# A small constant as a ninth row, one relu remainder moved behind a balancing chain, and six tile scalings on ScalarE

## The reference

```python
logits = x @ w_gate
logits = logits - logits.max()
P = np.exp(logits)
for _ in range(8):
    P /= P.sum(1, keepdims=True) + 1e-09     # over the 8 experts of a token
    P /= P.sum(0, keepdims=True) + 1e-09     # over all 2304 tokens of an expert
    P *= N / E
out = np.zeros((N, D), dtype=np.float32)
for e in range(E):
    h = np.maximum(x @ w1[e], 0.0)
    ye = h @ w2[e]
    out += P[:, e:e + 1] * ye
```

## Time and profile before

| what | value |
|---|---|
| median of three runs | 1865.8 us |
| the profiled execution's own time | 1865.84 us |
| its span, first to last instruction | 1864.0 us |
| PE, share of the span busy | 99% |
| VectorE, ScalarE, GpSimd busy | 58%, 44%, 55% |
| PE idle between 382 and 490 us (108.00 long, 101.09 busy) | 6.91 us |
| PE idle from 490 us to the end (1374.00 long, 1369.93 busy) | 4.07 us |

### The profile page before, as it was taken

One profiled execution on the slowest core, in us unless ns is written; L12 is line 12 of the kernel. 1 busy time (PEld: TensorE's weight loads), 2 busy tenths in 40 slices (PEclk: granted clock), 3 DMA queues, 4 the chain that ended last, 5 costly groups with the idle time before them and its releaser, 6 DMA issues.

```text
span 1864.0 us, 28112 instructions
## 1 busy us (share of the span) xinstructions
PE 1841.2 (99%) x10255; PEld 1594.7 (86%) x10255; DVE 1072.5 (58%) x1846; ACT 815.6 (44%) x1410; POOL 1027.8 (55%) x720
## 2 busy tenths in 40 slices
PE   8999999999999999999999999999999999999999
PEld 4677777788899999999999999999999999999998
DVE  8877777778845554556455545554555455545553
ACT  8777767533333333334333343333333333333331
POOL 0223226476666666665776666666665666666661
PEclk9999999999999999999999999999999999999999
DMA  7763552111111211112211211122122111111110
GB/s 245 221 150 87 131 144 54 46 68 69 47 69 69 69 68 69 68 69 99 72 69 69 70 68 70 69 69 70 70 94 76 69 69 68 70 69 69 69 51 34
DMA packets 44163, 152.57 MB, mean 82 GB/s; under 512 B 9594, under 2 KB 18042, under 8 KB 29710
## 3 DMA queue, kind: packets, MB, share of 16 engines
q1 hardware_dynamic: 44046, 151.04, 25.1%
HBM read 135.69 MB, written 15.34 MB: 81 GB/s over the span
## 4 chain that ended last, share of the span: by engine, by line
PE 94%; DVE 4%; ACT 1%; issue 1%; DMA 0%; DVEq 0%; SPq 0%; ACTq 0%
PE banks L673 13%; PE banks L674 13%; PE banks L672 13%; PE banks L640 12%; PE banks L644 12%; PE banks L642 12%; PE banks L555 4%; PE banks L516 3%; PE banks L498 3%; PE banks L464 2%; PE banks L499 2%; DVE h_lo L1173 1%; PE banks L581 1%; DVE routing L1129 0%; PE banks L526 0%
## 5 line engine op out<-in xcount | busy, mean ns | idle before, releaser
L1283 POOL TENSOR_TENSOR w_lo<-stage,w_hi 128x1024 fp32r<-128x1024 f32 (+1 forms) x288 | 646.8, 2260 | 539.8 <-ACT w_hi L842 538.1
L1167 DVE TENSOR_TENSOR u<-p_copy,banks 128x384 f32<-128x384 f32 x192 | 106.4, 554 | 632.3 <-PE banks L644 632.2
L674 PE MATMUL banks<-w_hi,h_lo 128*128 128x512 f32 x1152 | 450.1, 391 | 0.0
L673 PE MATMUL banks<-w_lo,h_hi 128*128 128x512 f32 x1152 | 449.9, 391 | 0.0
L672 PE MATMUL banks<-w_hi,h_hi 128*128 128x512 f32 x1152 | 448.9, 390 | 0.0
L1173 DVE SCALAR_TENSOR_TENSOR h_lo<-corner,h_hi 128x384 fp32r<-128x384 f32 x384 | 408.1, 1091 | 0.0
L889 ACT ACTIVATE h_hi<-corner 128x384 fp32r<-128x384 f32 x384 | 196.6, 526 | 272.5 <-DVE corner L1167 269.3
L640 PE MATMUL banks<-x_hi,w_hi 128*128 128x384 f32 x896 | 301.1, 336 | 4.9 <-DVE u L1167 2.4
L644 PE MATMUL banks<-x_hi,w_lo 128*128 128x384 f32 x896 | 300.2, 335 | 0.0
L842 ACT ACTIVATE w_hi<-stage 128x1024 fp32r<-128x1024 f32 (+1 forms) x288 | 271.7, 974 | 7.9 <-POOL stage L1277 7.9
L878 ACT ACTIVATE p_copy<-banks 128x384 f32<-128x384 f32 x96 | 47.3, 492 | 503.7 <-PE banks L644 503.7
(11 more groups left out here) (135 smaller groups left out, 2501.4 us busy)
## 6 DMA issues: line engine op xcount, KB each, us to landing
stage<-in_expert_w SPq DMA_DIRECT2D x96, 1024.0 KB, 4.7
raw<-in_qk SPq DMA_DIRECT2D x32, 576.0 KB, 7.2
bias_scratch<-bias_out SPq DMA_DIRECT2D x36, 288.0 KB, 2.8
bias<-bias_scratch SPq DMA_DIRECT2D x16, 288.0 KB, 2.8
v_main<-in_v SPq DMA_DIRECT2D x16, 256.0 KB, 2.7
bias<-bias_scratch SPq DMA_DIRECT2D x16, 256.0 KB, 3.8
out<-total SPq DMA_DIRECT2D x4, 768.0 KB, 3.9
out<-total SPq DMA_DIRECT2D x6, 256.0 KB, 2.0
```

The lines of the kernel that those rows point to most:

```text
L673: pe.matmul(dst, h_hi[:, g % 2, f, tokens], lo[:, f], start=False, stop=False)
L674: mm = pe.matmul(dst, h_lo[:, g % 2, f, tokens], hi[:, f], start=False, stop=fp == FPAIRS - 1 and f == 1)
L1167: dve.tensor_tensor(out, other, bank, op).then_inc(combined, 1)
L1283: pool.tensor_tensor(lo, of, hi.bitcast(F32), ALU.subtract).then_inc(w_split, 1)
```

## The change

There are four edits. First, a buffer `weighed` of nine rows of 18 takes the place of `routing`, which becomes a view of its first eight rows; the ninth row holds 1e-9, written once at the start. The sums over the experts now add nine rows, and the separate addition of the constant goes. Second, in periods with a total at place 4 (2, 3, 5 and 6) split 3 moves from ahead of the second chain to behind it. Third, the six scalings of the first expert's tiles move from VectorE to ACT, behind its last weight rounding of period 7; ACT waits there for the last column scaling (`balanced`). Fourth, the spreading of the largest logit moves on PE from behind token block 5 of period 1 to behind block 4.

```diff
-        routing = sb("routing", [P, E, TOK])
+        weighed = sb("weighed", [P, E + 1, TOK])
+        routing = weighed[:, 0:E]
...
-        TOP_ALL = (1, 5)
+        TOP_ALL = (1, 4)
...
+            def scale_first(j):
+
+                act.wait_ge(balanced, 1)
+                act.wait_ge(y_added, j + 1)
+                act.activation(total[:, j, :], total[:, j, :], ACT.Copy,
+                               scale=tile_weight(0, 0, j)).then_inc(first_scaled, 1)
...
+                if g == TOTALS[-1][0]:
+                    for j in range(TJ):
+                        scale_first(j)
...
             dve.memset(ones[:], 1.0).then_inc(ones_set, 1)
+            dve.memset(weighed[:, E], EPS).then_inc(eps_set, 1)
...
                 if k == 0:
+                    dve.wait_ge(eps_set, 1)
                     dve.wait_ge(exp_ready, 1)
-                link(dve.tensor_reduce(sums[:], routing[:].rearrange("p e c -> p c e"), AX_X, ALU.add))
-                link(dve.tensor_scalar(sums[:], sums[:], EPS, None, ALU.add))
+                link(dve.tensor_reduce(sums[:], weighed[:].rearrange("p e c -> p c e"), AX_X, ALU.add))
                 link(dve.reciprocal(inverse[:], sums[:]))
...
+                if k < ITERS - 1:
+                    link(scaled_columns)
+                else:
+                    scaled_columns.then_inc(balanced, 1)
...
-            def scale_first(j):
-
-                dve.wait_ge(y_added, j + 1)
-                dve.tensor_scalar(total[:, j, :], total[:, j, :], tile_weight(0, 0, j), None,
-                                  ALU.mult).then_inc(first_scaled, 1)
...
-                if g == 2 * FPAIRS - 2:
-                    scale_first(j)
...
                     if expert == 1:
+                        dve.wait_ge(balanced, 1)
                         dve.wait_ge(first_scaled, j + 1)
...
-                split_hidden(g, 3)
+                if (g, 4) not in TOTALS:
+                    split_hidden(g, 3)
                 add_tile(g - 1, 2)
                 for j in range(3, TJ):
                     read_side(g, j)
                     add_tile(g - 1, j)
+                if (g, 4) in TOTALS:
+                    split_hidden(g, 3)
```

More of the change, by code:

```diff
@@ L232, in bass_attention_moe @@
         first_scaled = sem("first_scaled")
+        balanced = sem("balanced")
+        eps_set = sem("eps_set")
         top_all = sem("top_all")
@@ L312, in first_low, with tile_weight @@
             return x_lo_first[:, k] if k < EARLY else x_lo_rest[:, k - EARLY]
+        def tile_weight(p, e, j):
+            return routing[:, e, TJ * p + j:TJ * p + j + 1]
         def high_part(p, k):
@@ L908, in place_logits @@
                 turned = banks[:, TURNED_BANK, :]
-                to = routing[:].rearrange("p e (j q) -> p q j e", q=T // P)
+                to = routing.rearrange("p e (j q) -> p q j e", q=T // P)
                 first = turned[:, 0:3 * P].rearrange("p (q j r) -> p q j r", q=T // P, r=C)
@@ L937, in _ @@
                     act.wait_ge(top_neg, 1)
-                    act.activation(routing[:], routing[:], ACT.Exp, bias=top[:, 1:2]).then_inc(exp_ready, 1)
+                    act.activation(routing, routing, ACT.Exp, bias=top[:, 1:2]).then_inc(exp_ready, 1)
                 if after == 1:
@@ L1104, in largest_logit @@
                 dve.wait_ge(logit_ready, 3)
-                dve.tensor_reduce(top[:, 0:1], routing[:].rearrange("p e c -> p (e c)"), AX_X,
+                dve.tensor_reduce(top[:, 0:1], routing.rearrange("p e c -> p (e c)"), AX_X,
                                   ALU.max).then_inc(top_ready, 1)
@@ L1124, in sinkhorn_rows @@
                 if k == 0:
+                    dve.wait_ge(eps_set, 1)
                     dve.wait_ge(exp_ready, 1)
-                link(dve.tensor_reduce(sums[:], routing[:].rearrange("p e c -> p c e"), AX_X, ALU.add))
-                link(dve.tensor_scalar(sums[:], sums[:], EPS, None, ALU.add))
+                link(dve.tensor_reduce(sums[:], weighed[:].rearrange("p e c -> p c e"), AX_X, ALU.add))
                 link(dve.reciprocal(inverse[:], sums[:]))
-                link(dve.tensor_tensor(routing[:], routing[:], over_experts(inverse[:]), ALU.mult))
-                dve.tensor_reduce(col_part[:], routing[:], AX_X, ALU.add).then_inc(col_ready, 1)
+                link(dve.tensor_tensor(routing, routing, over_experts(inverse[:]), ALU.mult))
+                dve.tensor_reduce(col_part[:], routing, AX_X, ALU.add).then_inc(col_ready, 1)
             def keep_totals(k):
@@ L1136, in keep_totals, with sinkhorn_columns @@
                 dve.wait_ge(totals_kept, k + 1)
-            def sinkhorn_columns():
+            def sinkhorn_columns(k):
                 link(dve.reciprocal(col_sum[:], col_sum[:]))
-                link(dve.scalar_tensor_tensor(routing[:], routing[:], float(N / E),
-                                              col_sum[:].unsqueeze(2).broadcast_to([P, E, TOK]), ALU.mult, ALU.mult))
+                scaled_columns = dve.scalar_tensor_tensor(routing, routing, float(N / E),
+                                                          col_sum[:].unsqueeze(2).broadcast_to([P, E, TOK]),
+                                                          ALU.mult, ALU.mult)
+                if k < ITERS - 1:
+                    link(scaled_columns)
+                else:
+                    scaled_columns.then_inc(balanced, 1)
             def read_side(g, j):
@@ L1152, in read_side @@
                     keep_totals(k)
-                    sinkhorn_columns()
+                    sinkhorn_columns(k)
                     if k < ITERS - 1:
                         sinkhorn_rows(k + 1)
-            def scale_first(j):
-                dve.wait_ge(y_added, j + 1)
-                dve.tensor_scalar(total[:, j, :], total[:, j, :], tile_weight(0, 0, j), None,
-                                  ALU.mult).then_inc(first_scaled, 1)
-            def tile_weight(p, e, j):
-                return routing[:, e, TJ * p + j:TJ * p + j + 1]
             def combine(out, bank, other, op):
```

## The result

The changed kernel takes 1856.85 us (median of 5 runs, 1855.81 to 1857.31) against 1865.8 us before: a ratio of 0.9949, with a 95% interval of 0.9935 to 0.9964. The profiled execution took 1856.01 us, with a span of 1854.2; before, 1865.84 and 1864.0.

A forecast was written before the change was run, and what follows sets the result against it. PE, busy 99% of the span, was taken as the bound: 7.8 us of printed waits plus 0.4 for spacing less 0.9 of new waits gives 7.3, so 1865.84 - 7.3 = 1858.5 us; range 1857.2 to 1861.0.

The forecast's parts named there:

- The ninth row: First chains of periods with totals: dropping the addition makes `col_part` early, removing four PE waits, 2.9 us.
- The rival in which the multiplication inherits both waits: First chains: multiplication also waits for GpSimd's second remainder, `col_part` stays late; gain 3.4, 1862.4 us; chance 0.07.
- The moved split: Split 3 behind the second chain: totals are read by 448.0, before product 0 is due at 449.0; 2.2 us go.
- The three waits for the totals: PE's product 0 waiting for the totals to be read; 2.2 us in all, claimed to go.
- The new wait for `u2`: Product 3 at the starts of periods 6 and 7 waits 0.45 us each, from 0 to at most 1.6.
- The rival with `u2` as the new bound: Second chains meet one more short GpSimd instruction; new waits about 1.5 us each, 1860.6 us; chance 0.12.
- The six scalings: Moved to ACT's idle time before `p_copy`, 4 to 4.5 us at no cost; period 8's `u2` wait of 2.4 us goes.
- The earlier spreading: VectorE copies the largest logit while PE does block 5; product 0's wait of 0.3 us goes.
- The layout: Rival: shifted buffers make matmuls read half a per cent slower, costing 17 us, 1876 us; chance 0.04.
- Spacing shows 0.04 to 0.1 more per wait than the printed idle time; for nine waits I add 0.4.: Term of the sum for PE's removed waits: 0.4 us of gain beyond the 7.8 us printed.
- 7.8 printed: PE's printed waits in the balancing stretch, 382 to 491 us: 2.9 + 2.2 + 2.4 + 0.3 us, all claimed to go.

The follow-up runs named there:

- the last version: Changed kernel with split 3 of periods 2, 3, 5, 6 behind the next `u2`, and split 0 behind corner 3 from period 3: 1855.75 us, ratio 0.9947.

## Why the prediction was right, and where it fell short

**The ninth row: right.** `col_part` was put at 445.5; it ends at 441.91, which with the 3.6 us saved up to there is the same. The four waits for it are gone (three of them by this edit, as the run without it showed; in period 2 the earlier spreading alone does as much), and the longer sum costs 0.04 us (0.45 for 0.41) where 0.05 stood. The rival in which the multiplication inherits both waits is out: the multiplication ended 0.17 us behind the first remainder. So the waiting VectorE operation did get in between two GpSimd instructions, as the addition did before.

**The moved split: right, and its price right in sum only.** The three waits for the totals are gone. The new wait for `u2` came where it was put, behind the order of operations that was written out. Its size was 0.45, twice. It measured 0.61 printed and 0.90 by the starts of the matmuls around it in period 6 (448.15 to 449.39, less the 0.34 that the same pair takes without a wait before, 453.88 to 454.22), and 0.22 with nothing printed in period 7: 1.1 instead of 0.9 in all. That the sum is close is luck: the one is double, the other half. In period 6 `u2` ended as forecast (449.04, which with the 3.6 us is 452.64, for 452.6), but PE came to product 0 0.2 us sooner than forecast (445.18 with the 3.6 is 448.78, for 449.0), since the waits ahead of it had cost more than printed, and the wait itself costs 0.3 more than printed. The rival with `u2` as the new bound (1.5 each) is out.

**The six scalings: right, and dearer than needed.** I took 4 to 4.5 us; they took 3.78, 0.63 each, and left `p_copy` 2.10 us of room. The Trainium skill (ScalarE: Activation LUTs, section "What ACT_TABLE_LOAD costs") gives 186 ns and 0.833 ns an element for such an instruction, 93 ns more for a scale read from memory, and 93 ns of overlap with the next: for six of 512 elements an estimate of 3.77 us from that page, and the trace agrees with 3.78.

**The earlier spreading: right**, 0.34 for 0.3, though it also changed the order of VectorE and GpSimd in period 2, which was not foreseen. **The layout: out**; both means of the earlier trace rows are unchanged to the nanosecond.

**The step that failed is "Spacing shows 0.04 to 0.1 more per wait than the printed idle time; for nine waits I add 0.4."** The waits and the paths were right; this term of the sum was far too small, and with it the gain. The starts of the rows show about 0.24 more per wait, not 0.04 to 0.1. At the totals' matmul it is 0.92 for 0.68. At product 0 of period 6 the starts are 1.64 us apart before,

```profile
449.46 0.39 PE L674 MATMUL banks<-w_hi,h_lo 128*128 128x512 f32 x1
...
451.10 0.34 PE L642 MATMUL banks<-x_lo_first_r,w_hi 128*128 128x384 f32 x1
```

and 0.40 after (444.95 to 445.35), so 1.24 for a printed 1.00. In period 8 it is 2.66 for 2.39. The step went wrong because it took 0.35, from 441.03 to 441.38, as the spacing without a wait. That place was itself a wait met as PE arrived, on the combination of a corner, as the weight load of that matmul shows:

```profile
441.38 0.30 PEld L720 LDWEIGHTS banks<-col_part,ones 128*128 128x128 f32 x2 [0.39 <-DVE corner L1167]
```

Without a wait the spacing is 0.23 (443.34 to 443.57), and the matmul behind the totals also follows later when they waited: 0.21 (448.01 to 448.22 of the trace of before) for 0.14 (443.57 to 443.71).

The sum as measured: 7.8 printed; 8 x 0.24 = 1.9 on top (the spreading's wait shows none); 0.4 for the totals at block 0 of periods 6 and 7, which had been met just in time and now are early; 0.15 at product 0 of period 4, where nothing was printed either (416.70 to 417.24 in the trace of before, 0.54 us, for 0.39 after); less 1.1 of new waits. That makes 9.15 us, against 9.16 in the stretch, and 1865.84 less 9.15 is 1856.7, against 1856.85 measured. By the prediction's own numbers the two errors are 2.05 us on the hidden part (2.45 for 0.4) and -0.2 on `u2`; its range had allowed 0.4 for the first. The 0.4 for the two places is worked out from the starts of their matmuls in the two traces. It came back with the split left where it was, together with other waits; no run took it alone.

Open is why product 0 of periods 6 and 7 comes later in the last version, and whether that version is 1 us faster than the changed kernel in whole time, as its stretch says: the intervals are too wide for it.

## What to carry to other kernels

When waits of a full engine go, count them by the starts of the instructions on either side, against a place where the signal is long there, and not by the printed idle time: here each wait was worth about 0.24 us more than printed, and some of the price stood where nothing was printed at all. Where two engines exclude each other an instruction at a time, an operation taken off the chain is worth the instruction that it would have met (1.65 us in the run that put the addition back), not its own 0.18 us, and nothing where the chain has room even so, as in period 2. Ask what the moved operation now stands ahead of: the split that left the totals' path came into that of `u2`. An empty list of waits does not mean that nothing is waited for: look at the weight loads too.

## What the runs showed of the hardware

- A wait on a weight load that is met as PE arrives cost 0.23 to 0.26 us with no idle time printed (five more reductions, periods 3 and 5); with the signal some 0.3 us ahead of the matmul it cost nothing (four more).
- One idle time of PE of 2.29 us was followed by a mean granted clock of 0.64 over 4.8 us (0.50 in 3.0 of them), one of 2.39 us in another kernel by 1.00.
- A VectorE operation that had to wait for GpSimd got in behind one GpSimd instruction although the next followed at once: the multiplication ended 0.17 us behind the first weight remainder.
- Six copies of 128x512 from buffer to buffer with a scale per partition took 3.78 us on ScalarE beside busy VectorE and GpSimd, and nothing in the row stretched.
